# Loads of q, k, v and bias, taken apart by heads and placed behind earlier bias stores

## The reference, cut to what matters

```python
# q, k, v: (B=4, H=8, S=576, D=64)
scores = q @ k^T / sqrt(D)                                   # (B, H, S, S)
psi_rel = log1p(abs(pos_i - pos_j))
psi_i = log1p(max(pos_i, 1))
bias = relu((psi_rel / psi_i) * w1 + b1) @ w2                # (S, S, H), hidden 32, same for every batch
attn = softmax(scores + bias.transpose(2, 0, 1))             # over the last axis
x = (attn @ v), heads side by side                           # (2304, 512)
h = max(x @ moe_w1, x @ moe_w2, x @ moe_w3)                  # (2304, 768)
y = h @ moe_w_out                                            # (2304, 512)
g = clipped square of (y @ moe2_w_in)                        # (2304, 2048)
out = g @ moe2_w_out                                         # (2304, 512)
```

## Time and profile before

| | |
|---|---|
| median of 3 runs | 1026.89 us (1025.89 to 1028.06) |
| profiled execution, its time | 1028.29 us |
| profiled execution, its span | 1026.5 us |
| mean granted clock of PE | 0.992 |
| PE busy | 994.7 us (97%) |
| DVE, ACT, POOL busy | 503.6, 490.7, 295.8 us |

### The profile page before, as it was taken

One profiled execution on the slowest core, in us unless ns is written; L12 is line 12 of the kernel. 1 busy time (PEld: TensorE's weight loads), 2 busy tenths in 40 slices (PEclk: granted clock), 3 DMA queues, 4 the chain that ended last, 5 costly groups with the idle time before them and its releaser, 6 DMA issues.

```text
span 1026.5 us, 20413 instructions
## 1 busy us (share of the span) xinstructions
PE 994.7 (97%) x7608; PEld 865.4 (84%) x7608; DVE 503.6 (49%) x1176; ACT 490.7 (48%) x1023; POOL 295.8 (29%) x506
## 2 busy tenths in 40 slices
PE   6959999999999999999999999999999999999998
PEld 3547767776767999999999999889989989899897
DVE  8946667667683231313232327754454444544543
ACT  8948788778783321212121225543343443433433
POOL 1049888888873700000000336700000000000000
PEclk9979999999999999999999999999999999999999
DMA  5872534425312400000000113200000000000000
GB/s 142 265 222 57 151 73 107 124 50 155 93 40 64 131 33 1 1 0 0 0 0 0 42 62 92 94 8 25 1 31 0 0 31 0 31 0 0 32 1 32
DMA packets 96043, 56.10 MB, mean 55 GB/s; under 512 B 64224, under 2 KB 81632, under 8 KB 95968
## 3 DMA queue, kind: packets, MB, share of 16 engines
q1 hardware_dynamic: 95872, 55.11, 19.0%
q10 hardware_dynamic: 96, 0.00, 0.0%
HBM read 39.46 MB, written 15.63 MB: 54 GB/s over the span
## 4 chain that ended last, share of the span: by engine, by line
PE 73%; DVE 1%; issue 0%; POOL 0%; ACT 0%; ACTq 0%; DVEq 0%
PE ps L1078 42%; PE ps L1137 20%; PE ps L1105 7%; PE ps L1029 2%; PE ps L977 1%; PE ps L990 1%; DVE s_sb L796 0%; PE ps L1004 0%; POOL probs L518 0%; PE ps L953 0%; DVE p_t L810 0%; DVE x_lo L851 0%; DVE row_min L796 0%; ACT o_sb L747 0%; DVE xT L817 0%
## 5 line engine op out<-in xcount | busy, mean ns | idle before, releaser
L1078 PE MATMUL ps<-x_hi,w_all 128*128 128x384 f32 x1632 | 437.8, 336 | 1.2 <-ACT ta L693 1.2
L1078 PEld LDWEIGHTS ps<-x_hi,w_all 128*128 128x128 f32 x1632 | 296.8, 188 | 7.2 <-DVE xT L817 1.7
L1078 PE MATMUL ps<-x_lo,w_all 128*128 128x384 f32 x816 | 273.2, 335 | 0.0
L1137 PE MATMUL ps<-w_all,g_hi 128*128 128x512 f32 x576 | 179.9, 393 | 0.0
L1078 PEld LDWEIGHTS ps<-x_lo,w_all 128*128 128x128 f32 x816 | 153.2, 188 | 3.9
L538 POOL TENSOR_TENSOR w_all<-raw,w_all 128x256 fp32r<-128x256 f32 x100 | 77.6, 807 | 273.8 <-ACT w_all L667 273.8
L796 DVE CUSTOM_DVE_ANT_0 s_sb<-ps,bias_h 128x576 f32<-128x576 f32 (+1 forms) x160 | 114.8, 753 | 80.3 <-PE ps L977 55.3
L602 ACT ACTIVATE probs<-s_sb,row_min 128x576 f32<-128x576 f32 (+1 forms) x160 | 122.2, 770 | 6.8 <-DVE row_min L796 6.8
L518 POOL TENSOR_SCALAR probs<-probs,row_inv 128x576 f32<-128x576 f32 (+1 forms) x160 | 121.3, 768 | 13.7 <-DVE row_inv L826 12.6
L1137 PEld LDWEIGHTS ps<-w_all,g_hi 128*128 128x128 f32 x576 | 106.2, 188 | 19.5 <-issue 1.2
L1137 PE MATMUL ps<-w_all,g_lo 128*128 128x512 f32 x288 | 113.9, 395 | 0.0
(11 more groups left out here) (85 smaller groups left out, 1327.4 us busy)
## 6 DMA issues: line engine op xcount, KB each, us to landing
bias_scratch<-p_t SPq DMA_DIRECT2D x36, 296.0 KB, 3.8
raw<-in_moe_w_out SPq DMA_DIRECT2D x22, 256.0 KB, 3.1
bias_h<-bias_scratch SPq DMA_DIRECT2D x16, 288.0 KB, 4.2
raw<-in_moe_w SPq DMA_DIRECT2D x18, 256.0 KB, 3.0
out<-o_sb SPq DMA_DIRECT2D x18, 256.0 KB, 2.1
q_in<-in_q SPq DMA_DIRECT2D x32, 128.0 KB, 2.4
bias_h<-bias_scratch SPq DMA_DIRECT2D x16, 256.0 KB, 3.2
v_in<-in_v SPq DMA_DIRECT2D x32, 128.0 KB, 2.4
```

Source lines behind the costliest of these rows:

```text
L1078: last = pe.matmul(ps[:, bank, 0:BLK], w[:, at:at + P], x[:, kt, :], start=(kt == 0 and n == 0), stop=(kt == KT - 1 and n == 2))
L1137: last = pe.matmul(ps[:, O_BANK + t, :], g[:, ft % 4, t * P:(t + 1) * P], w[:, wout_d(ft):wout_d(ft) + DM], start=(opens and i == 0), stop ...
```

## The change

SP's stream is put in another order; the transfers themselves are the same, and no other engine's program is touched. `load_q`, `load_k` and `load_v` get an argument h and issue one head. In the bias stage one head of one input at most stands behind a store: q of group 1 behind stores 2 and 3, k of group 1 behind 4 and 5, bias tile 0 behind 14 and 15, q and k of group 2 behind 16 to 19 (with the wait on `lo_ok` now behind store 16, not 22), bias tile 1 behind 22 and 23, v of group 0 behind 24 and 25, bias tile 2 behind 30 and 31. Behind store 35 only bias tiles 3 and 4 are left. `load_qk` of later groups issues q and k of head 0, and then of head 1, where it issued q of both heads and then k of both.

```diff
-            def load_q(i):
+            def load_q(i, h):
+
                 par = i % 2
-                for h in range(2):
-                    x = q[i % B, 2 * (i // B) + h, :, :]
-                    sp.dma_start(q_in[:, par, 0:T, h, :],
+                x = q[i % B, 2 * (i // B) + h, :, :]
+                sp.dma_start(q_in[:, par, 0:T, h, :],
+                             x[0:MAIN, :].rearrange("(t p) d -> p t d", t=T)).then_inc(qk_in[par], 16)
+                sp.dma_start(q_in[0:HALF, par, T, h, :], x[MAIN:S, :]).then_inc(qk_in[par], 16)
...
-                load_q(i)
-                load_k(i)
-
-            def load_v(i):
-
-                if i >= 2:
+                for h in range(2):
+                    load_q(i, h)
+                    load_k(i, h)
+
+            def load_v(i, h):
+
+                if i >= 2 and h == 0:
                     sp.wait_ge(o_ps, 2 * (i - 2) + 2)
...
             for s in range(NSUP):
                 store_bias(s)
-                if s == 8:
-                    load_q(1)
-                if s == 14:
-                    load_k(1)
-                if s == 22:
+                if s in (2, 3):
+                    load_q(1, s - 2)
+                if s in (4, 5):
+                    load_k(1, s - 4)
+                if s % 8 in (6, 7) and 14 <= s < NSUP - 4:
+                    first_bias(s % 8 - 6, s // 8 - 1, s // 8 * 8)
+                if s == 16:
                     sp.wait_ge(lo_ok, NT)
-                    load_q(2)
-                if s == 26:
-                    load_k(2)
-                if s in (11, 12):
-                    first_bias(s - 11, 0, s - 3)
-                if s in (NSUP - 3, NSUP - 2):
-                    first_bias(s - NSUP + 3, 1, 2 * P // SUP)
-            for t in range(2, T):
+                if s in (16, 17):
+                    load_q(2, s - 16)
+                if s in (18, 19):
+                    load_k(2, s - 18)
+                if s == 24:
+                    sp.wait_ge(staged_zero, 1)
+                if s in (24, 25):
+                    load_v(0, s - 24)
+            for t in range(T - 1, NT):
                 for h in range(2):
-                    first_bias(h, t, (t + 1) * P // SUP)
-            sp.wait_ge(staged_zero, 1)
-            load_v(0)
-            for h in range(2):
-                first_bias(h, T, NSUP)
+                    first_bias(h, t, min((t + 1) * P // SUP, NSUP))
...
                 if i:
-                    load_v(i)
+                    for h in range(2):
+                        load_v(i, h)
```

More of the change, by code:

```diff
@@ new lines, in load_q, with load_k @@
+                sp.dma_start(q_in[:, par, 0:T, h, :],
+                             x[0:MAIN, :].rearrange("(t p) d -> p t d", t=T)).then_inc(qk_in[par], 16)
+                sp.dma_start(q_in[0:HALF, par, T, h, :], x[MAIN:S, :]).then_inc(qk_in[par], 16)
+            def load_k(i, h):
+                par = i % 2
+                x = k[i % B, 2 * (i // B) + h, :, :]
+                if h == 0:
+                    sp.dma_start(k_in[:, par, 0:T, 0, :],
+                                 x[0:MAIN, :].rearrange("(t p) d -> p t d", t=T)).then_inc(qk_in[par], 16)
+                    sp.dma_start(k_in[0:HALF, par, T, 0, :], x[MAIN:S, :]).then_inc(qk_in[par], 16)
+                else:
+                    halves = x[0:MAIN, :].rearrange("(t r p) d -> r p t d", t=T, r=2)
+                    sp.dma_start(k_in[HALF:P, par, 0:T, 1, :], halves[0]).then_inc(qk_in[par], 16)
+                    sp.dma_start(k_in[0:HALF, par, 1:NT, 1, :], halves[1]).then_inc(qk_in[par], 16)
+                    sp.dma_start(k_in[0:HALF, par, 0, 1, :], x[MAIN:S, :]).then_inc(qk_in[par], 16)
@@ L344, in load_qk @@
                     sp.wait_ge(lo_ok, NT * (i - 1))
-                load_q(i)
-                load_k(i)
-            def load_v(i):
-                if i >= 2:
-                    sp.wait_ge(o_ps, 2 * (i - 2) + 2)
-                for h in range(2):
[L353 to L357, removed]
+                for h in range(2):
[3 more added lines that the diff above has]
+                if i >= 2 and h == 0:
+                    sp.wait_ge(o_ps, 2 * (i - 2) + 2)
+                x = v[i % B, 2 * (i // B) + h, :, :]
+                sp.dma_start(v_in[:, i % 2, h, 0:T, :],
+                             x[0:MAIN, :].rearrange("(t p) d -> p t d", t=T)).then_inc(vv_in[i % 2], 16)
+                sp.dma_start(v_in[h * HALF:(h + 1) * HALF, i % 2, h, T, :],
+                             x[MAIN:S, :]).then_inc(vv_in[i % 2], 16)
             def load_bias(hp, h, t):
```

2 lines of the change are left out of this document (removed).

## The result

| | before | changed |
|---|---|---|
| median of 20 runs each | 1027.97 us (1025.89 to 1029.56) | 1025.70 us (1023.70 to 1027.40) |
| ratio of medians, 95% interval | | 0.9978 (0.9972 to 0.9985) |
| profiled execution, time and span | 1028.29 and 1026.5 us | 1023.70 and 1021.9 us |

The change gains 2.3 us (1.5 to 2.9 by the interval), a little over the 0.2% that can be told. The forecast was 8.0 us, with 4.2 to 9.3 us in the range. The profiled execution of the changed kernel is the fastest of its 20. A second one, taken with the first experiment, took 1025.34 us (span 1023.5 us) and is nearer to the usual case. Both are used here.

The account below looks back on a forecast made before the run. Late bias loads in SP's queue were taken to bound the start of attention, PE the rest. 8.44 us at slot 5, less 0.2 for tile 4 and 0.2 for POOL, gave 8.0: 1026.89 to 1018.9 us, range 1017.6 to 1022.7.

Parts of the forecast that it names:

- What bounds the kernel now: Between 51 and 77 us, bias loads late in SP's queue hold DVE 7.0 us and PE's clock falls; elsewhere PE-bound.
- Slots of 2.65 us: Attention slots 0 to 4 take 2.65 us each at full clock; slot 5 starts at 69.71 us, 8.44 us earlier.
- That ... its end, slot 0 at 56.46 us, stays: DVE sets the bias stage, so its end, slot 0's start at 56.46 us, does not move.
- slower: copies wait for stores: Rival, chance 0.04: in the bias stage, late stores hold buffers and stall ACT, then PE and DVE; 1029 us or more.
- T = 58.7 us: In SP's queue, store 35 is out at 58.7 us (11.29 + 43.4 + 4), where it was 62.72 us.
- v and bias tile 2 moved ahead: SP's list: early v gains nothing, four issues some 2.2 us; tile 2, issued between 50 and 56 us, costs nothing.
- The clock falls all the same: Rival, chance 0.15: PE's clock falls, slots 2 to 5 at 3.47 us; gain 5.2 us, time 1021.7 us.
- Bias tile 4: Just fits slot 4, costing 0.2 us; rival, chance 0.14: 3.9 to 4.1 us late, gain about 4.2, time 1022.7 us.
- Everything passes through: From slot 5 on PE is the bound to the end, so the 8.0 us shift passes through whole.

Follow-up runs that it names:

- the first experiment: The changed kernel itself, unaltered, timed and profiled a second time: 1025.34 us, ratio to before 0.9978.
- v_back: The changed kernel with v of group 0 back behind bias tile 3: 1024.59 us, ratio to before 0.9968.
- the kernel with T at 58.1 us and nothing held: The changed kernel with v behind bias tile 3, q and k of group 2 issued by ACT, and 11 buffers: 1024.32 us, ratio to before 0.9969.
- issues_added: The changed kernel with one more transfer of 64 bytes behind each of stores 16 to 25: 1030.55 us, ratio to before 1.0023.
- act_k2: The changed kernel with v behind bias tile 3 and k of group 2 issued by ACT: 1023.17 us, ratio to before 0.9952.

## Why the prediction was wrong, step by step

- **What bounds the kernel now**: right in the main. The waits, the hole at slot 1, the late queue of SP and the fallen clock were what they seemed. (One row was misread, without use in the sum: the highest DMA share in the earlier trace rows is in the second slice, 8, and not in the third, 7.) Reading them as one hole was wrong: tile 1 was the first of four tiles behind the same list, and removing its wait alone moved nothing (0.9996).
- **Slots of 2.65 us**: right where nothing waits. v_back and the kernel with fewer bytes have 2.72 to 2.74 us for slots 0 to 2, 0.08 us more than I had.
- **"That ... its end, slot 0 at 56.46 us, stays"**: wrong, 1.35 and 2.04 us. I counted a backlog of at most 4.9 us behind store 25, under the 5.5 us from which copies are held. Store 26 actually went out some 9 us after ACT had its data. The mechanism stood among the rivals as "slower: copies wait for stores"; it came, but cost 1.4 us at slot 0 in the first profile, 2.0 at slot 0 and 1.7 at slot 1 in the second, and not 8 or more.
- **T = 58.7 us**: the step that failed most. The busy part of the count was right (51.1 us from store 0 to store 35, less 7.7 of waiting for ACT, is 43.4 us, as I had). The waiting that stays was put at 4 us and was 7.7, and that is the whole error of T. SP waited 3.3 us between 23 and 31 us, behind the loads of stores 2 to 5 and ahead of those of group 2, and some 2 us after 31 us. Early issues use up early waiting, but nothing of a list in order can use a wait that comes behind them. I also had 18 issues leave the late, crowded part; nine of them, group 1's, had stood behind stores 8 and 14, and only group 2's nine were late. T was 62.4 us, and bias tile 3, for which I had 64.7 at the worst, landed at 68.2 us.
- **v and bias tile 2 moved ahead**: of v I said that its early landing gains nothing and put its four issues at 2.2 us. They had stood in the wait for store 35, where they were nearly free; behind stores 24 and 25 they took 3.3 us of the scarce queue. Putting v back gave 0.8 to 1.0 us by the medians, within the noise. Of tile 2 I said "Cost nothing". Its loads were issued at 57.8 to 60.5 us and not between 50 and 56, and its second head was 0.39 us late in the first profile.
- **The clock falls all the same**: it did, in both profiles, at 0.15 in my chances. It fell after PE had stood still for 2.3 us (second profile, 58.0 to 60.3 us) and after 1.3 us of standstill with little before (first), so the rival was no alternative to late stores but came with them. In the second profile two slots at the low clock are 3.47 us apart, 0.75 us more than the 2.72 at the full one, and nothing else held them. In the first the clock was low while slot 3 waited for tile 3 in any case. What it costs in the usual execution stays open.
- **Bias tile 4**: not the wait; in the first profile tile 3 was, one tile earlier, since T was late. The rival did ask what happens if T stays at 62.7 us, but priced tile 4 alone (gain 4.2 us); tile 3 with such a T, and the copies that late stores hold, were left out of it. The stores' median landing rose from 3.8 to 4.6 and 4.4 us. By the Trainium skill's figure quoted in the prediction (DMA: Bandwidth & Descriptors, Latency and other measured facts) the estimate was 4.9 us; the runs lie between.
- **Everything passes through**: right within 0.3 us.

So the forecast of 8.0 us failed on two terms: T (58.7 us forecast, 62.4 measured), and slot 0, which was to stay and came 1.4 to 2.0 us late. With T late, bias tile 3 or the held copies took the rest, by execution.

What stays open: why 11 buffers alone made the changed kernel lose its gain, and what the clock's fall costs by itself, as each run that removed a wait changed the clock too. Even the kernel with T at 58.1 us and nothing held gained 3.3 us, so a right T by itself need not have made the forecast right.

## What to carry to other kernels

A queue that issues in order is a resource with a time of its own. Count its issues in the stretch before the deadline, and don't subtract waits that lie elsewhere. Before a transfer is moved earlier, ask what it stood behind: one that sits in a wait is free, and any other place for it may not be. When the first of several loads behind one list is late, look at when the last one can land; that, and not the first hole, limits what the change can gain.

## What the runs showed of the hardware

- A bare transfer of 64 bytes held SP for 0.59 us, as long as a store of 296 KB (0.52 to 0.6 us; both in the lines of issues_added above). Single issues took 1.1 to 1.8 us, on SP and on ACT alike, mostly with a DMA share of 0.9 or more (a store of 1.40 us in the changed kernel at 56.1 us; 1.77 us on ACT in act_k2, share 1.03). But one of 1.79 us stood in a stretch with a share of 0.65 (issues_added, 41.5 us), so the share alone doesn't say which.
- Two issues on POOL stood for 9.17 and 22.36 us while DVE worked without gaps, and ended within 0.5 us of the start of a gap of DVE's and of the end of its last hidden activation. The Trainium skill (DMA: Bandwidth & Descriptors, SWDGE vs HWDGE vs iDMA) says that POOL writes its descriptors into SBUF, from which DVE locks it out in one of its modes. The two long issues agree with such a lock-out, but six more went through between 24.61 and 28.69 us in 0.55 to 0.92 us each, with DVE busy throughout, from 25.30 us on with the same kind of instruction. So something is missing from that account, and no run here changed DVE's mode to show it.
